# Forty-two matrix products of constants at the head of an attention and two feed-forward kernel

## The reference

```
scores = scale * q_rot @ k_rot.T            # 4 batches x 8 heads, 576 positions, head size 64
scores = scores - max(scores, axis=-1)      # q_rot, k_rot: rotary position code applied
attn   = exp(scores) / (sum(exp(scores)) + 1e-9)
x      = attn @ v                           # as 2304 tokens x 512
h = x @ w_in;   x = (h - tanh(h)) @ w_out        # 512 -> 2048 -> 512
h = x @ w_in2;  y = (h * sigmoid(h)) @ w_out2    # 512 -> 2048 -> 512
```

## Time and profile before

| | |
|---|---|
| median of 3 runs | 1104.58 us (1103.09 to 1106.67) |
| the profiled execution | 1107.88 us, span 1106.0 us |
| PE busy | 1064.7 us (96%) |
| DVE, ACT, POOL busy | 435.3, 412.1, 282.8 us |
| mean granted clock of TensorE | 0.991 |
| PE's first matmul | 11.59 us into the span |
| PE idle in the first 62 us, by what ended it | ACT 11.6, `negmax` 4.8, `hm` 2.6, transfer of maxima 2.1 us |

### The profile page before, as it was taken

One profiled execution on the slowest core, in us unless ns is written; L12 is line 12 of the kernel. 1 busy time (PEld: TensorE's weight loads), 2 busy tenths in 40 slices (PEclk: granted clock), 3 DMA queues, 4 the chain that ended last, 5 costly groups with the idle time before them and its releaser, 6 DMA issues.

```text
span 1106.0 us, 18105 instructions
## 1 busy us (share of the span) xinstructions
PE 1064.7 (96%) x7404; PEld 997.6 (90%) x7404; DVE 435.3 (39%) x696; ACT 412.1 (37%) x760; POOL 282.8 (26%) x127
## 2 busy tenths in 40 slices
PE   3889999989999999999999999999999999999998
PEld 2879888879999999999999999899989989899897
DVE  5556666656252323232232333523223232322322
ACT  2557776666722323223232322323223232232322
POOL 6667897966470000000000015700000000000000
PEclk9999999999999999999999999999999999999999
DMA  5445455453151000000000004200000000000000
GB/s 194 161 140 157 143 147 179 143 160 84 38 188 52 1 1 0 0 0 0 0 0 0 0 0 152 77 1 28 0 0 28 0 28 0 0 28 0 28 0 29
DMA packets 36368, 60.54 MB, mean 55 GB/s; under 512 B 15712, under 2 KB 18016, under 8 KB 34400
## 3 DMA queue, kind: packets, MB, share of 16 engines
q1 hardware_dynamic: 36320, 59.87, 17.0%
HBM read 50.46 MB, written 4.79 MB: 50 GB/s over the span
## 4 chain that ended last, share of the span: by engine, by line
PE 82%; DMA 8%; SPq 3%; POOL 3%; DVE 2%; ACT 1%; issue 1%; ACTq 0%; POOLq 0%; DVEq 0%
PE ps L722 35%; PE ps L741 18%; PE ps L736 17%; DMA inverse_sums<-rinv 4%; PE ps L592 3%; PE ps L556 2%; PE ps L586 2%; DMA R<-inverse_sums 2%; DMA sums<-ev 1%; PE ps L496 1%; PE ps L622 1%; SPq L282 1%; DVE hm L919 1%; POOL xT L412 1%; PE ps L546 1%
## 5 line engine op out<-in xcount | busy, mean ns | idle before, releaser
L722 PE MATMUL ps<-xs_h,win_l 128*128 128x384 f32 x768 | 258.6, 337 | 1.4 <-DVE xs_l L979 1.4
L722 PE MATMUL ps<-xs_h,win_h 128*128 128x384 f32 x768 | 257.6, 335 | 0.0
L722 PE MATMUL ps<-xs_l,win_h 128*128 128x384 f32 x768 | 257.1, 335 | 0.0
L884 ACT ACTIVATE g_h<-ps 128x384 fp32r<-128x384 f32 x192 | 94.4, 492 | 306.1 <-PE ps L741 135.1
L878 ACT ACTIVATE act<-ps 128x384 f32<-128x384 f32 x192 | 94.5, 492 | 247.7 <-PE ps L722 247.6
L722 PEld LDWEIGHTS ps<-xs_h,win_l 128*128 128x128 f32 x768 | 144.2, 188 | 7.5 <-issue 3.9
L722 PEld LDWEIGHTS ps<-xs_l,win_h 128*128 128x128 f32 x768 | 144.2, 188 | 3.5
L722 PEld LDWEIGHTS ps<-xs_h,win_h 128*128 128x128 f32 x768 | 144.1, 188 | 0.0
L919 DVE TENSOR_REDUCE hm<-ps 128x2 f32<-128x576 f32 x144 | 108.5, 756 | 63.4 <-PE ps L496 56.8
L736 PE MATMUL ps<-g_h,wout_h 128*128 128x384 f32 x384 | 128.3, 334 | 0.0
L736 PE MATMUL ps<-g_h,wout_l 128*128 128x384 f32 x384 | 128.3, 334 | 0.0
(11 more groups left out here) (86 smaller groups left out, 1619.6 us busy)
## 6 DMA issues: line engine op xcount, KB each, us to landing
raw<-qk SPq DMA_DIRECT2D x15, 1152.0 KB, 5.9
w_stage<-w_in SPq DMA_DIRECT2D x8, 1024.0 KB, 5.0
w_stage<-w_out SPq DMA_DIRECT2D x8, 1024.0 KB, 5.2
v<-vfull SPq DMA_DIRECT2D x16, 384.0 KB, 4.1
R<-inverse_sums SPq DMA_DIRECT2D x32, 144.0 KB, 3.1
out<-ostage SPq DMA_DIRECT2D x5, 768.0 KB, 3.5
vr<-vin SPq DMA_DIRECT2D x16, 192.0 KB, 3.2
ev<-ev SPq DMA_DIRECT2D x16, 144.0 KB, 2.3
```

The source lines that it names most:

```text
L722: last = mm(o, w[g][:, kk, c:c + 128], x[:, kk, :], start=(n == 0), stop=(n == 11))
L884: nc.scalar.activation(g_h[f % 2][:, :], ps[:, 4 + f % 4, 0:TN], ACT.Copy, scale=(1.0, 0.5)[L]).then_inc(s_gh, 1)
```

## The change

PE gets a helper that multiplies a 128 x 128 stationary part of `w1` by all 256 columns of `w1`, `count` times, into the first 256 columns of PSUM bank `OB`. It is called three times: 24 passes behind the wait for the constants and ahead of the first row score, 8 behind the last row score of pair 0, and 10 behind the transposes of `negmax`. The products are never read: the first product of v into `OB` overwrites them. No wait and no increment is added, and no other engine's stream changes.

```diff
+            def idle_passes(count):
+
+                for _ in range(count):
+                    mm(ps[:, OB, 0:256], w1[:, 0, :], w1[:, :, :], start=True, stop=True)
+
             pe.wait_ge(s_cst, 8)
+            idle_passes(24)
             for j in range(7):
                 row_scores((0, j), (XB, 2)[j % 2])
             row_scores((0, 8), 2)
             row_scores((0, 7), XB)
             row_scores((0, 9), 2)
+            idle_passes(8)
             pe.wait_ge(s_id, 16)
             max_transpose(0, XB).then_inc(s_tm, 1)
+            idle_passes(10)
             for n in range(PAIRS):
```

## The result

| | before | changed |
|---|---|---|
| median of 20 runs | 1104.72 us | 1107.86 us |
| lowest and highest | 1101.28, 1107.64 | 1105.73, 1111.81 |
| the profiled execution, its span | 1107.88, 1106.0 us | 1111.81, 1109.9 us |

A forecast was written before the change was run, and what follows sets the result against it. PE is busy 96% of the span, but in the head it waits for others, and `v_high(1)` at 33.48 us walls off its lead. Only 0.31 us of ACT's idle time is won: 1104.6 - 0.3 = 1104.3 us, range 1101.8 to 1106.6.

The forecast's parts named there:

- the sum: Total of the terms: 0.31 us less, up to 0.1 us of delay swallowed by 0.46 us of slack; 0.3 us less.
- the slower one: Rival: passes take 0.3 to 0.44 us each and delay transposes and first scores; 1105.4 to 1107.9 us, chance 0.09.
- three signs of being wrong: In the changed profile: `v_high(1)` earlier than 33.3 us, passes slower than 0.27 us, or transposes before 39.5 us.
- 24 passes: Ahead of the first row score: end at 8.8 to 9.3 us, cost nothing with 2.3 us of room, gain taken as 0.
- 8 passes: Behind pair 0's row scores: run from 18.08 to 19.79 or 19.93 us, cost 0 to 0.07 us.
- 10 passes: Behind the transposes: 2.1 to 2.3 us from about 20.0, cost 0 to 0.1 us; 0.1 together with the 8.
- The clock: PE's clock in the head: up at some 22 to 24 us, not 30; not rising earlier was a rival, chance 0.12.
- The wall: `v_high(1)` on ACT stays at 33.48 us, so PE waits its lead away before 35.98; only 0.31 us won behind.
- Carried to the end: Rival: no wall at `v_high(1)`, PE's lead of 1.2 to 2.6 us lives on; 1102.0 to 1103.4 us, chance 0.12.
- the slow stretch behind 40.5 us goes: Rival: PE's slow clock after 40.5 us, costing 1.1 us, vanishes; 1103.2, or 1100.9 us with a full lead, chance 0.05.
- Passes slower than a stream: Rival: passes writing one PSUM place and reloading weights take 0.3 to 0.44 us; decides from about 0.27, chance 0.09.

The follow-up runs named there:

- e7: 24, 6 and 7 full passes in place of the change's 24, 8 and 10, against the kernel before: 1104.94 us, ratio 1.0032.
- e15: Kernel before plus 12 full and 103 16-column passes ahead of the row scores, 6 full behind them, 7 behind the transposes (256 instructions): 1104.83 us, ratio 1.0013.
- e12: Kernel before plus 110 16-column passes ahead of the row scores and the full 8 and 10 at their places (256 instructions): 1102.85 us, ratio 0.9999.

## Why the prediction was wrong

**The step that failed** is the one behind the sum: "What is late next is all released by that ... from there the order and the waits are those of before." I had costed 42 products as time on PE and had shown that nearly all of it is taken up. I had not costed them as 84 instructions of code, a term that the sum puts at nothing without a reason. The runs show that it is not nothing: instructions that take next to no time cost as much as the passes, 2.6 ± 0.2 us over the kernels that shift PE's code by part of a block (3.1 us by the medians in the changed one), more than eight times what I had been adding up, and 0.7 ± 0.4 us where the shift is filled up to a whole block. The road from there to the end, through transfers that the packets meet or slow stretches of the clock, is open. None of my rivals held this; the slower one had its 0.09 for another mechanism, and the right answer stood outside of my range, at 1107.86 against 1106.6. None of my three signs of being wrong came up either: `v_high(1)` was not before 33.3 us, no pass took 0.27, and no transposes came before 39.5. The line that could have warned me was on the page of before, the queue of code with its 33 packets.

**24 passes** cost PE's products nothing, right: they ended at 8.17 us, and alone they are at 1.0013 (0.9993 to 1.0034), which leaves open whether their 48 instructions cost anything. I had counted no gain for the row scores, right as well: the clock had gone again before them, and a row score takes 0.61 us with the start of the group, as before. (In the profile of e7 the set ended at 9.23 us and the clock was still up at 11.50: the first group took 0.53 us for 0.85 and the second came 0.2 us sooner, as I had it for that case, and no more.) The 0.7 us by which the head came late was a load's, as the 11.47 us in the kernel with the 24 passes alone show.

**8 passes** were mis-sized. I took 0.21 to 0.23 us for a pass, and they took 0.25. The transposes started 0.35 us late (20.21 in the kernel without the 24 passes, 19.86 before), where I had 0 to 0.07. **10 passes**: 2.17 us there and 2.50 in the changed kernel, where `scores(0, 0)` started 2.64 us behind the transposes instead of 2.41: 0.23 us late for my 0.1. Together 0.35 to 0.6 us for 0.1, all of it swallowed.

**The clock** rose at 23.7 us, inside the forecast of 22 to 24, and at 21.4 to 24.0 in the four other profiles with at least 8 and 10 full passes behind the row scores. With 6 and 7, which leave PE a pause of 0.34 us before `scores(0, 0)`, it did not rise that early: it was back at 29.5 and 31.2 us (e7 and e15; 30.3 and 31.6 in the two of before). A window of e7:

```profile
23.80:25.50 1.70, 1.55 (x12) 0.98 (x8) 1.53 (x3) 1.35 (x4) 1.70 (x1) 0.50 0.00 0
```

So these two kernels can't say what an earlier clock is worth. That it would fall again at 27.1 us in the changed kernel I had not seen; no price of it shows, for the wall was there.

**The wall** held. `v_high(1)` started at 33.4 to 35.1 us over all profiles, 21.7 to 23.3 behind the first row score, and no earlier where PE had won time (21.9 in the kernel with the 8 and 10 passes, as in the kernel before), and the new wait of PE for `low` was there (1.02 us at 35.88). The 0.31 us that I saw as won behind the wall came out as 0.45 in the kernel with the 8 and 10 passes, between two single executions. Filled up to a block (e12, 0.9999 with 0.9981 to 1.0017) the full passes show no gain that can be measured. 0.3 us would look like that, and so would nothing: the size of the forecast gain is not shown.

**Carried to the end** and **the slow stretch behind 40.5 us goes** didn't happen; the stretch stands in the changed kernel too (granted clock 0.50 from 40.8 us on). The 1.1 us that I took for the price of such a stretch is what comes out of the comparison of the profiles above, too. **Passes slower than a stream** had its deciding point at 0.27 us a pass, and 0.25 stayed below it. Doubling the passes behind the row scores (1.0028) shows that it would not have come to much: the transposes of pair 1 came at 42.06 us, 1.6 late, and the end not measurably later than with the single number.

## What to carry to other kernels

Before you cost an edit as nothing because its engine waits there anyway, count its instructions as code: in this kernel a shift of PE's code by less than a block cost more than all the time of the added products. Test it with the same number of instructions that take next to no time, and once filled up to a whole block, 256 here (254 by the records); if the two differ, what you measure is the shift and not your idea. An effect of 0.25% needs many executions of each kernel, and its own control. And warming TensorE ahead of a stretch that another engine's chain bounds bought nothing that could be measured here: find the wall first.

## What the runs showed of the hardware

- PE's code comes in packets of 16384 bytes, on average 254 recorded instructions apart, in a DMA queue that the page lists apart from the data's (q8: 33 packets, 0.54 MB). 36 instructions more, of 18 products of 16 columns, changed this kernel by 1.0041, 1.0036 and 1.0022 in three groups; 256 instructions more, in five kernels, by 0.9999 to 1.0017.
- 24 products of 256 columns raised the clock while PE had nothing else to do (1.00 from 6.70 to 10.00 us, and the set ended at 8.17 for the 9.8 that 0.25 us each would give), and it was at 0.50 in the window from 10.10, after 2 us without a product. It rose again at 23.7 us and fell at 27.1; in the window of 3.2 us between, PE had been busy for 1.66, with no pause longer than 1.36.
- A printed 1.00 in the head is not always the full pace. In the kernel before, the windows print 1.00 for 24 to 28 us, where six products of the scores take 0.72 us from their start to the next group's (26.74 to 27.46). In the changed kernel they take 0.72 us under 0.50 (27.56 to 28.28) and 0.40 us under 1.00 (24.37 to 24.77). The first record of the clock in the trace is at 30.33 us before and at 6.64 us changed, and the row scores, at the same pace in both, stand under 0.50 in the second.
- Products of 128 rows and 256 columns that load their stationary part each time take 0.25 us at a granted clock of 0.50 (8 from 18.90 to 20.90 us), 17% more than the pace of 288 columns with 64 rows (0.24 us a pair) gives for 256.
